# The second pair's broadcast sums, and when the DMA queue goes on to the third pair's q and k

## What is computed

```python
scores = scale * np.matmul(q, k.transpose(0, 1, 3, 2))
log_f = np.log(np.clip(f, 0.0001, 1.0))
cum = np.cumsum(log_f, axis=-1)
decay = cum[:, :, :, None] - cum[:, :, None, :]
scores = np.where(causal, -1000000000.0, scores + decay)
scores = scores - np.max(scores, axis=-1, keepdims=True)
attn = np.exp(scores)
attn = attn / (np.sum(attn, axis=-1, keepdims=True) + 1e-09)
x = np.matmul(attn, v)                  # then, as [2304, 512]:
x = (silu(rmsnorm(x) @ w_gate) * (rmsnorm(x) @ w_val)) @ w_out
x = silu(x @ w_in) @ w_out2
```

## Time and profile before

| | |
|---|---|
| median of three runs | 987.19 us |
| lowest, highest run | 986.37, 988.2 us |
| profiled execution, its own time | 987.51 us |
| span of its records | 985.8 us |
| PE busy | 978.8 us (99%) |
| DVE, ACT, POOL busy | 643.9, 454.6, 342.3 us |
| mean rate of the DMA queues | 195 GB/s |

### The profile page before, as it was taken

One profiled execution on the slowest core, in us unless ns is written; L12 is line 12 of the kernel. 1 busy time (PEld: TensorE's weight loads), 2 busy tenths in 40 slices (PEclk: granted clock), 3 DMA queues, 4 the chain that ended last, 5 costly groups with the idle time before them and its releaser, 6 DMA issues.

```text
span 985.8 us, 16401 instructions
## 1 busy us (share of the span) xinstructions
PE 978.8 (99%) x5807; PEld 889.8 (90%) x5807; DVE 643.9 (65%) x1265; ACT 454.6 (46%) x975; POOL 342.3 (35%) x318
## 2 busy tenths in 40 slices
PE   8999999999999999999999999999999999999998
PEld 5777776899999999999999999989989899898996
DVE  6777789688758797788682787704837148371441
ACT  6877787545254235245242343523615236152341
POOL 6777755603302563235334243120221202212022
PEclk9999999999999999999999999999999999999999
DMA  7667565276826666569479477342563425634212
GB/s 200 209 189 240 157 186 160 97 288 232 302 108 258 265 223 228 200 258 346 160 277 338 187 258 270 125 171 90 192 256 117 168 100 189 254 113 171 107 34 95
DMA packets 74144, 192.68 MB, mean 195 GB/s; under 512 B 8464, under 2 KB 38928, under 8 KB 67920
## 3 DMA queue, kind: packets, MB, share of 16 engines
q1 hardware_dynamic: 74064, 191.64, 54.6%
HBM read 150.12 MB, written 41.49 MB: 194 GB/s over the span
## 4 chain that ended last, share of the span: by engine, by line
PE 94%; DVE 3%; ACT 1%; DMA 1%; issue 1%; SPq 0%; POOL 0%; ACTq 0%; DVEq 0%; POOLq 0%
PE banks L1878 19%; PE banks L1880 19%; PE banks L1879 19%; PE banks L2011 7%; PE banks L2010 7%; PE banks L2009 7%; PE banks L1768 5%; PE banks L1804 5%; PE banks L1720 4%; PE banks L1780 1%; DMA cum_b<-cum_dram 1%; DVE wu L1396 0%; DVE scratch L1567 0%; PE banks L1733 0%; DMA cum_dram<-zeros 0%
## 5 line engine op out<-in xcount | busy, mean ns | idle before, releaser
L1878 PE MATMUL banks<-xb,wu 128*128 128x384 f32 x864 | 289.0, 334 | 0.0
L1880 PE MATMUL banks<-xb,wu 128*128 128x384 f32 x864 | 288.7, 334 | 0.0
L1879 PE MATMUL banks<-xb,wu 128*128 128x384 f32 x864 | 288.6, 334 | 0.0
L856 POOL TENSOR_TENSOR wd<-stage_d,wd 128x512 fp32r<-128x512 f32 x84 | 118.2, 1413 | 470.2 <-ACT wd L1057 470.2
L1878 PEld LDWEIGHTS banks<-xb,wu 128*128 128x128 f32 x864 | 162.2, 188 | 0.4 <-issue 0.2
L1879 PEld LDWEIGHTS banks<-xb,wu 128*128 128x128 f32 x864 | 162.2, 188 | 0.2
L1880 PEld LDWEIGHTS banks<-xb,wu 128*128 128x128 f32 x864 | 162.2, 188 | 0.0
L1139 ACT ACTIVATE scratch<-scratch 128x384 f32<-128x384 f32 x144 | 75.3, 523 | 113.0 <-DVE scratch L1525 51.2
L1148 ACT ACTIVATE hid_main<-scratch 128x384 fp32r<-128x384 f32 x144 | 72.2, 517 | 117.8 <-DVE scratch L1567 117.8
L1057 ACT ACTIVATE wd<-stage_d 128x512 fp32r<-128x512 f32 x84 | 51.6, 629 | 138.2 <-PE banks L2011 100.3
L1574 DVE TENSOR_TENSOR hid_main<-scratch,hid_main 128x384 fp32r<-128x384 f32 x144 | 88.3, 627 | 40.6 <-ACT hid_main L1148 36.3
(11 more groups left out here) (190 smaller groups left out, 1718.3 us busy)
## 6 DMA issues: line engine op xcount, KB each, us to landing
wu<-kept SPq DMA_DIRECT2D x48, 1792.0 KB, 9.9
stage_d<-w SPq DMA_DIRECT2D x84, 256.0 KB, 2.8
kept<-ws SPq DMA_DIRECT2D x14, 1024.0 KB, 5.3
kept<-wu SPq DMA_DIRECT2D x12, 768.0 KB, 4.5
qk_raw<-qk_t SPq DMA_DIRECT2D x14, 576.0 KB, 3.4
cum_b<-cum_dram SPq DMA_DIRECT2D x30, 256.0 KB, 4.3
kept<-xb SPq DMA_DIRECT2D x6, 1024.0 KB, 5.3
kept<-ws SPq DMA_DIRECT2D x8, 768.0 KB, 5.1
```

The costliest lines, as they stand in the source:

```text
L856: nc.gpsimd.tensor_tensor(wd[:, d % 2, 1, :], stage_d[:, d % 2, :], f32(wd[:, d % 2, 0, :]), ALU.subtract).then_inc(wd_split, 1)
L1878: nc.tensor.matmul(dst, w_hi_part, m_hi, start=start, stop=False)
L1879: nc.tensor.matmul(dst, w_hi_part, m_lo, start=False, stop=False)
L1880: return nc.tensor.matmul(dst, w_lo_part, m_hi, start=False, stop=stop)
```

## The change

SyncE waits, after issuing the three DMAs of `load_cum(1)`, until all three have landed, and only then goes on to `load_qk(2)` and all that follows.

```diff
             sp.wait_ge(cum_out, 16)
             load_cum(1)
+            sp.wait_ge(cum_in[1], 48)
             load_qk(2)
             load_v(0)
             load_cum_rest(1)
```

## The result

The changed kernel takes 988.8 us in the median of 18 runs (987.39 to 991.71); the kernel before, in 18 runs, 986.81 us (986.36 to 988.2). The ratio is **1.0022, with a 95% interval of 1.0015 to 1.0029**: about 2 us slower. The runs of the changed kernel are also spread more widely, over 4.3 us against 1.8.

The account below looks back on a forecast made before the run. PE, busy 978.8 of 985.8 us, was taken to bound the kernel; v landing at 21.7 us instead of being read at 20.83 adds 0.9 us, broadcast gain included, to the median 987.2: 988.0 us, range 986.2 to 989.6.

Parts of the forecast that it names:

- its own sign: In the changed profile: wrong if the third broadcast takes under 4.5 us, PE has no wait at v, or waits again later.
- Do the broadcasts land earlier: Broadcasts of pair 1: only traffic issued behind could slow them; 0.2 us gain, bounds none to 1.9, PE using at most 0.98.
- g: Forecast gain in the landing of pair 1's third broadcast: 0.2 us, from 5.1 to 4.9 us.
- Rival B: Queueing behind the broadcasts slowed them: landing 1 us or more earlier, PE loses most of 0.98 us idle, 986.2 us; chance 0.12.
- rule of ring order: DMA engines consume one queue's descriptors in ring order, so the broadcasts gain 0 and the sum is below 0.2 us higher.
- How long v then takes: v of pair 0, issued at 17.4 us, takes 4.3 us (3.1 to 4.7 in later pairs), landing at 21.7 us.
- Rival C: SyncE refills the queue in one go, v takes 5.7 us, PE waits at `values(0, 0)` until 23.3: +2.5, 989.7 us; chance 0.12.
- the prediction's own sum: PE at v of pair 0: broadcasts land 15.75 us, v issued 17.4, lands 21.7 against 20.83 wanted: 0.9 us later.
- The other readers: DVE and POOL in pairs 1 to 3: later transfers in time or tight, nothing charged; slowest masks of pair 2 cost 0.7 us.

Follow-up runs that it names:

- the two profiles above: First profile of the changed kernel, execution 987.39 us, and a second from rerunning it without edit, median 988.47 us, ratio 1.0019.
- the three later profiles: Three more profiles of the changed kernel, no edit, one run each: 988.02, 987.98 and 988.02 us.
- the second order: Against the changed kernel: v of pair 0 ahead, broadcasts of pair 2 right after q and k of pair 2, no added wait; 986.95 us, ratio 1.0001.
- the first attempt with the transfers in the readers' order: Against the changed kernel: v of pair 0 ahead of the wait, broadcasts of pair 2 right after q and k of pair 2; 987.24 us, ratio 1.0002.

## Why the prediction came out as it did

The median, 988.8 us, lies in the range given (986.2 to 989.6), the direction was right and so was the wait that was to decide: PE waits for v of pair 0 at `values(0, 0)`. By its own sign the prediction was wrong in another part: the third broadcast was not to take under 4.5 us, and it took 4.0 to 4.3. The size was too small: +0.9 us was forecast and about +2 measured, at the very edge of what I called no change, and the chances (0.88 for within 0.2%) leaned too hard on the inside of it. That the forecast came as near as it did is in part luck: two of its terms were off by about 1 us in opposite directions. Point by point:

- **"Do the broadcasts land earlier": g = 0.2 us. Wrong.** The gain is 1.0 us: 4.0 us in four of five profiles of the changed kernel (4.3 in the first) against 5.0 and 5.1 without the wait, and 4.9 with q and k alone behind. No large packet of q and k starts before 14.8 us, and I took the 26 small ones left by then for a tail of no account. But the third broadcast lands with its last packet, and its last ones start among the large packets, as late as 15.4 to 15.6 us. And I had taken the best of 13 later pairs (4.9) as the price of an undisturbed broadcast. But in all 13 other transfers are issued right behind, as here; none of those rows showed the case wanted. Rival B, which had the mechanism ("by the queueing of what follows"), was given 0.12 for that reason. Its price was wrong besides: it had v there by 20.7 us and yet took off most of the 0.98 us, to 986.2; with v read at 20.7 instead of 20.83, B comes out at about no change. The Trainium skill's rule of ring order (DMA: Bandwidth & Descriptors, queues, rings and completion order) gave g = 0; the measurement decides against that reading of it. The rule speaks of each engine for itself, and the trace agrees only that no large packet started before 14.8 us; a DMA issued behind still delays a landing.
- **"How long v then takes": 4.3 us. Mis-sized.** 5.2 and 5.5 us in the two profiles above. By PE's start it is 5.7 to 5.9 in the three later profiles (issued at 15.60, 15.48 and 15.58, read at 21.30, 21.38 and 21.47). The later pairs were the wrong guide again. Rival C had 5.7.
- **The two errors nearly cancel, by luck.** With the measured terms the prediction's own sum reads: the broadcasts land at 10.89 + 4.0 = 14.9, v is issued 1.55 us after q and k, at 16.4, and lands 5.2 to 5.9 us later, at 21.6 to 22.3. That is 0.8 to 1.5 us after 20.83. The 19 runs of the changed kernel that are not at 0.998 have a mean of 988.4 us, 1.25 over the mean of 77 runs of the kernel before (987.1; the first three comparisons have 78, and one of 5497 us is left out). The forecast counted from one profile of before, and of all 14 profiles that one has the latest sums (first broadcast at 9.91 us, the others 8.62 to 9.84), and the longest wait of PE for the broadcasts. Counted from the issue of the first broadcast, PE reads v after 10.8 to 10.9 us in the four profiles that issue q and k right behind the broadcasts (the kernel before, v ahead without the wait, the wait after q and k, the second order), and after 12.1 to 12.5 in the five of the changed kernel. That is 1.1 to 1.7 us later, an estimate that holds the 1.25.
- **A term is missing: most likely the clock.** 10 of the 29 runs are at 0.998, with a mean of 990.3 us, 2.0 over the others; that adds 10/29 x 2.0 = 0.7 us to the mean, and the two parts make the 1.9 us between the means. Of the kernel before it is one of the 75 runs whose clock is on record, and one of 11 of the first attempt with the transfers in the readers' order. That the lower clock costs these 2.0 us is inferred: a longer wait for v could come together with it. I had seen a wait of 0.98 us without any effect on the clock and never asked what one twice as long would do.
- **"The other readers":** the broadcasts of pair 2 were forecast to reach POOL at 26 to 27 us, at no cost; they came at 26.3 and 26.9, at no cost to PE. Right, but only because PE was late itself: with v in time they cost 0.73 us. q and k of pair 3 came late for DVE by 0.83 us, called tight but in time; PE did not feel it.

## What to carry to other kernels

A wait put in front of a queue is paid by the first reader of what stands behind it, so list those readers with their slack before placing it; here the wait gained 1.0 us for one transfer and lost more on the next but one. When a reader is brought forward, the transfers after it come due in turn: the lead of 0.76 us was lost twice before the whole order followed the readers, and even then the gain of 0.35 us is not clear of the noise. And a price taken from rows is only as good as the likeness of their surroundings: ask what was issued behind a transfer too.

## What was not expected of the hardware

A DMA of 128 KB in short rows landed 1.0 us sooner (4.0 against 4.9 to 5.1 us) when nothing was issued behind it until it had landed, though 0.64 MB of packets, as much as the three broadcasts hold, were the only ones to start from 10.8 to 14.8 us; the last small ones started among large ones at 15.4 to 15.6 us. And v, 320 KB, took 3.2 us when it was issued 0.9 us before q and k had landed, and 5.0 to 5.9 in six profiles in which it was issued 1.55 us behind them. Which of the transfers behind v share in that was not tried. TensorE's clock went to 0.50 during an idle stretch of 2.6 us and stayed there for 6.8 us, 5.9 of them with PE at work again.
